# Attention, mixture of experts and feed-forward on one core: three tiles of the last stage taken into the last expert, and the first weight splits in other iterations

## The reference, cut to what matters

```python
# windowed attention, B=4, H=8, S=576, head size 64; window of 64 keys
scores = scale * q @ k.T, masked to 0 <= i - j < 64;  attn = softmax(scores);  x = attn @ v      # x: 2304 x 512
# mixture of experts: 8 experts, 512 -> 1024 -> 512, two per token
noisy = x @ w_gate + log1p(exp(x @ w_noise)) * noise
top2, weights = two largest of noisy, softmax over the two
for e in range(8):
    for k in range(2):
        mask = top2[:, k] == e
        h = maximum(x[mask] @ w1[e], 0)
        out[mask] += weights[mask, k] * (h @ w2[e])
# dense feed-forward, 512 -> 2048 -> 512
h = out @ w_in;  g = h * clip(h + 3, 0, 6) / 6;  result = g @ w_out
```

## Time and profile before

| | us |
|---|---|
| median of 3 runs (1078.79 to 1080.82) | 1079.85 |
| the profiled execution's own time | 1081.28 |
| its span, first to last instruction | 1079.5 |
| PE busy | 1010.3 (94%) |
| DVE, ACT, POOL busy | 418.8, 232.1, 414.5 |

### The profile page before, as it was taken

How to read it: one execution, slowest core, us unless ns; L and a number is a source line. 1 busy time by engine, 2 the same in 40 slices (tenths; PEclk the granted TensorE clock), 3 DMA queues, 4 the chain that set the end, 5 groups by cost and what they waited for, 6 DMA issues and landing times.

```text
span 1079.5 us, 20340 instructions
## 1 busy us (share of the span) xinstructions
PE 1010.3 (94%) x8098; PEld 895.0 (83%) x8099; DVE 418.8 (39%) x885; ACT 232.1 (22%) x537; POOL 414.5 (38%) x277
## 2 busy tenths in 40 slices
PE   6889847999999999999999976999999999999998
PEld 5657727998989999999999966898988988899897
DVE  3477764222213122222222134544545445444333
ACT  4547610111111111111111121111111111211111
POOL 3343469858291928375573817400100101000000
PEclk9989967999999999999999996999999999999999
DMA  8658447936171624435242313310110101100000
GB/s 198 159 140 214 147 161 260 319 123 203 57 224 65 186 100 157 144 106 195 85 159 79 123 63 126 89 30 30 42 48 19 39 29 39 49 1 1 30 1 30
DMA packets 105177, 115.21 MB, mean 107 GB/s; under 512 B 27552, under 2 KB 72608, under 8 KB 105120
## 3 DMA queue, kind: packets, MB, share of 16 engines
q1 hardware_dynamic: 86784, 74.04, 23.5%
q10 hardware_dynamic: 12576, 21.50, 5.7%
q0 software_dynamic: 5760, 18.88, 5.4%
HBM read 76.13 MB, written 38.27 MB: 106 GB/s over the span
## 4 chain that ended last, share of the span: by engine, by line
PE 88%; DVE 6%; issue 2%; SPq 1%; DMA 1%; POOL 1%; ACT 1%; ACTq 0%; DVEq 0%; POOLq 0%
PE PS L1459 21%; PE PS L1443 21%; PE PS L1560 19%; PE PS L1544 19%; PE PS L1328 2%; PE PS L1427 2%; PE PS L1307 1%; PE PS L1291 1%; PE PS L1248 1%; SPq L446 1%; DVE negmax L926 1%; PE PS L1533 1%; DMA k_raw<-in_k_dram 1%; PE PS L1340 1%; PE PS L1269 0%
## 5 line engine op out<-in xcount | busy, mean ns | idle before, releaser
L1459 PE MATMUL PS<-W,hs_room 128*128 128x512 f32 x960 | 246.8, 401 | 4.1 <-DVE hs_room L1071 4.1
L1443 PE MATMUL PS<-xs,W 128*128 128x256 f32 (+1 forms) x1536 | 249.0, 313 | 1.5 <-DVE xs L1065 1.5
L1443 PEld LDWEIGHTS PS<-xs,W 128*128 128x128 f32 x1536 | 239.5, 190 | 12.3 <-issue 2.4
L1560 PE MATMUL PS<-W,gs 128*128 128x512 f32 x864 | 217.4, 396 | 3.6 <-issue 2.5
L1544 PE MATMUL PS<-x2s,W 128*128 128x384 f32 x1152 | 218.9, 339 | 1.5 <-DVE x2s L1168 1.5
L1544 PEld LDWEIGHTS PS<-x2s,W 128*128 128x128 f32 x1152 | 203.4, 190 | 9.0 <-issue 1.9
L610 POOL TENSOR_TENSOR W<-stage,ones_f 128x1024 fp32r<-128x1024 f32 x76 | 144.7, 1903 | 166.9 <-PE PS L1459 156.2
L1459 PEld LDWEIGHTS PS<-W,hs_room 128*128 128x128 f32 x960 | 175.9, 190 | 37.9 <-DVE hs_room L1071 4.5
L1071 DVE SCALAR_TENSOR_TENSOR hs_room<-PS,hs_room 128x256 fp32r<-128x256 f32 (+1 forms) x128 | 62.8, 491 | 333.4 <-ACT hs_room L783 333.2
L1560 PEld LDWEIGHTS PS<-W,gs 128*128 128x128 f32 x864 | 160.9, 188 | 36.0 <-issue 5.8
L612 POOL TENSOR_TENSOR W<-stage,W 128x1024 fp32r<-128x1024 f32 x76 | 181.9, 2393 | 6.0
(11 more groups left out here) (134 smaller groups left out, 580.0 us busy)
## 6 DMA issues: line engine op xcount, KB each, us to landing
stage<-in_moe_w_dram SPq DMA_DIRECT2D x64, 512.0 KB, 4.4
x_in<-x_sorted ACTq DMA_DIRECT2D x40, 256.0 KB, 5.0
x_sorted<-zeros SPq DMA_DIRECT2D x8, 1280.0 KB, 7.5
y_sorted<-y_sb ACTq DMA_DIRECT2D x40, 256.0 KB, 2.1
vD<-in_v_dram SPq DMA_DIRECT2D x72, 64.0 KB
out_dram<-o_sb SPq DMA_DIRECT2D x18, 256.0 KB, 2.2
stage<-in_moe_w_in_dram SPq DMA_DIRECT2D x8, 512.0 KB, 3.9
stage<-in_moe_w_out_dram SPq DMA_DIRECT2D x8, 512.0 KB, 3.6
```

Source lines behind the costliest of these rows:

```text
L1443: last = nc.tensor.matmul(HP_[:, c % 2, 0:n], W[:, par, 0, b, at:at + P], xs[:, a, kd, rows], start=start, stop=(kd == KD - 1 and (a, b) = ...
L1459: last = nc.tensor.matmul(Y[:, first + t, :], hs[:, c % 2, a, t * P:(t + 1) * P], W[:, par, 1, b, c * DM:(c + 1) * DM], start=(c == 0 and ...
L1560: last = nc.tensor.matmul(OP[:, tt, :], gs[:, c % 2, a, tt * P:(tt + 1) * P], W[:, 1, c // FC, b, at:at + DM], start=(c == 0 and (a, b) == ...
```

## The change

Four edits.

- The order in the last expert. Its second part now also prepares tiles 0, 1 and 2 of the last stage: POOL gathers them as soon as blocks 0 to 2 of the last expert and everything older are stored; DVE mixes them after its c = 4, 5, 6; PE turns them after `hidden(5)`, `hidden(6)`, `hidden(7)` (`LAST_AT`); ACT and DVE split them behind that. The gathers of tiles 3, 4, 5 move ahead of POOL's splits of `w_out`. These three tiles always have their rows of the last expert in its blocks 0 to 2.
- The results of part 0, in every expert: DVE copies blocks 0 and 1 before `h_lo(0)` and block 2 behind it; ACT stores 0 and 1 after `h_hi(0)` and 2 after `h_hi(1)`.
- Buffers. `xs` and `x2s` are each two tensors now, laid so that the new ones use rooms that are free in time; `hidden2(0)` has a new wait (`more_moved`), since it writes where the branch of a sixth block would.
- Attention. `FIRST_AT` and `SPLIT_AT`: chunk 3 is loaded after iteration 7 instead of 5 and split in 9 instead of 7; chunk 4 is split in 13 instead of after the loop; later chunks follow.

```diff
+    LAST_AT = (5, 6, 7)
-    FIRST_AT = (2, 3, 4, 5, 7, 9, 11, 13)
-    SPLIT_AT = (4, 5, 6, 7)
+    FIRST_AT = (2, 3, 4, 7, 9, 11, 12, 13)
+    SPLIT_AT = (4, 5, 6, 9, 13)
...
-            split_first(QCH)
+            split_first(QCH + 1)
...
-            for c in range(QCH + 1, SCH):
+            for c in range(QCH + 2, SCH):
...
-            for j in range(BLOCKS):
-                pool.wait_ge(y_stored[j], 16 * (E + 1))
-            pool.wait_ge(more_stored, 16 * (MORE * E + 1))
-
...
+            for j in range(BLOCKS):
+                pool.wait_ge(y_stored[j], 16 * (E + 1) if j < PARTS[1][0] else 16 * E)
+            pool.wait_ge(more_stored, 16 * (MORE * (E - 1) + 1))
             for T in range(GT):
                 gather(T)
 
             expert_done(E - 1)
+            for j in range(PARTS[1][0], BLOCKS):
+                pool.wait_ge(y_stored[j], 16 * (E + 1))
+            pool.wait_ge(more_stored, 16 * (MORE * E + 1))
+            for T in range(GT, 2 * GT):
+                gather(T)
             for c in range(QCH, SCH):
                 pool.wait_ge(stage_full[c % STAGES], 16 * (2 * (E + 1) + 2))
                 split(1, c, (E + 1) * SCH + c - QCH, (E + 1) * SCH + c - QCH + 1)
-            for T in range(GT, TILES):
+            for T in range(2 * GT, TILES):
                 gather(T)
...
-                    if 1 <= c <= PARTS[0][1]:
-                        store_y(e, c - 1, base)
+                    for j in ((0, 1), (2,))[c] if c < 2 else ():
+                        store_y(e, j, base)
...
+                    if c in LAST_AT and last:
+                        x2_hi(LAST_AT.index(c), LAST_AT.index(c), 0)
...
+                move_y(e, 0)
+                move_y(e, 1)
                 for c in range(FC):
                     h_lo(e, 1, c)
-                    if c < PARTS[0][1]:
-                        move_y(e, c)
+                    if c == 0:
+                        move_y(e, 2)
                     if c in TURN_AT[1] and not last:
                         x_lo(e + 1, TURN_AT[1].index(c))
+                    if last:
+                        if c in LAST_AT:
+                            x2_lo(LAST_AT.index(c), LAST_AT.index(c), 0)
+                        if c + 1 in LAST_AT:
+                            mix(LAST_AT.index(c + 1), LAST_AT.index(c + 1))
...
+                        if part == 1 and c in LAST_AT and last:
+                            transpose_x2(LAST_AT.index(c), LAST_AT.index(c))
...
-            for tt in range(GT):
-                transpose_x2(tt, tt, OP[:, tt, :])
             pe.wait_ge(w_ready, SCH * (E + 1))
+            pe.wait_ge(more_moved, MORE * E + 1)
             hidden2(0, 0, 0)
```

More of the change, by code:

```diff
@@ L414, in if_more, with x_place @@
                     eng.sem_inc(signal, each * MORE)
+        def x_place(j, a):
+            part = 0 if j < PARTS[1][0] else 1
+            at = (j - PARTS[part][0]) * P
+            return xs[part][:, a, :, at:at + P]
         def unit(e, part, c):
@@ L1083, in move_y, with mix, x2_lo @@
                 nc.vector.tensor_copy(y_sb[:, j % 3], Y[:, j, :]).then_inc(y_moved, 1)
+            def mix(T, tt):
+                gi = T // GT if isinstance(T, int) else None
+                dve.wait_ge(g_full[tt], 32 * (gi if gi is not None else T[1]) + 32)
+                Tn = T if gi is not None else T[0]
+                nc.vector.tensor_scalar(ya[:, tt, :], ya[:, tt, :], gate[:, 0, bass.ds(Tn, 1)], None, ALU.mult)\
+                    .then_inc(mix_a, 1)
+                dve.wait_ge(mix_a, Tn + 1)
+                nc.vector.scalar_tensor_tensor(yb[:, tt, :], yb[:, tt, :], gate[:, 1, bass.ds(Tn, 1)], ya[:, tt, :],
+                                               ALU.mult, ALU.add).then_inc(x2_ready, 1)
+            def x2_lo(T, tt, par):
+                at = slice(tt * P, (tt + 1) * P)
+                dve.wait_ge(x2hi, T + 1)
+                nc.vector.tensor_tensor(x2s[par][:, 1, :, at], XTP.rearrange("p (k n) -> p k n", k=KD),
+                                        x2s[par][:, 0, :, at].bitcast(F32), ALU.subtract).then_inc(x2_split, 1)
             def more_block(e, t):
@@ L1199, in _ @@
                     .then_inc(out_ready, 1)
[L1200 to L1203, removed]
-            x2_lo(GT - 1, GT - 1, 0, OP[:, GT - 1, :])
             with dve.Fori(0, GPAIRS - 1) as gp:
@@ L1432, in hidden @@
                 first, blocks = PARTS[part]
-                rows, n = slice(first * P, (first + blocks) * P), blocks * P
+                n = blocks * P
                 if c == 0:
@@ L1442, in hidden @@
                     for a, b in PASSES:
-                        last = nc.tensor.matmul(HP_[:, c % 2, 0:n], W[:, par, 0, b, at:at + P], xs[:, a, kd, rows],
+                        last = nc.tensor.matmul(HP_[:, c % 2, 0:n], W[:, par, 0, b, at:at + P], xs[part][:, a, kd, :],
                                                 start=start, stop=(kd == KD - 1 and (a, b) == PASSES[-1]))
@@ L1498, in more_block, with transpose_x2 @@
                 last.then_inc(more_y, 1)
+            def transpose_x2(T, tt):
+                pe.wait_ge(x2_ready, T + 1)
+                pe.wait_ge(x2_split, T + 1)
+                for kd in range(KD):
+                    last = nc.tensor.transpose(XTP[:, kd * P:(kd + 1) * P], yb[:, tt, kd * P:(kd + 1) * P], ident[:])
+                last.then_inc(t2_full, 1)
             def expert(e, par, last=False):
@@ L1508, in expert @@
                         hidden(e, par, part, c)
-                        if c in TURN_AT[part]:
-                            j = TURN_AT[part].index(c)
-                            if part == 0:
-                                turn_x(e, PARTS[1][0] + j)
-                            elif not last:
-                                turn_x(e + 1, j)
+                        if part == 0 and c in TURN_AT[0]:
+                            turn_x(e, PARTS[1][0] + TURN_AT[0].index(c))
+                        if part == 1 and c in TURN_AT[1] and not last:
+                            turn_x(e + 1, TURN_AT[1].index(c))
+                        if part == 1 and c in LAST_AT and last:
+                            transpose_x2(LAST_AT.index(c), LAST_AT.index(c))
                         project(e, par, part, c - 1)
@@ L1526, in _ @@
             expert(E - 1, 1, last=True)
-            def transpose_x2(T, tt, bank=XTP):
-                pe.wait_ge(x2_ready, T + 1)
-                if bank is XTP:
-                    pe.wait_ge(x2_split, T + 1)
-                for kd in range(KD):
-                    last = nc.tensor.transpose(bank[:, kd * P:(kd + 1) * P], yb[:, tt, kd * P:(kd + 1) * P], ident[:])
-                last.then_inc(t2_full, 1)
             def hidden2(gi, c, par):
```

46 lines of the change are left out of this document (16 added, 30 removed).

## The result

The changed kernel takes 1068.68 us (median of 4 runs, 1066.27 to 1070.30) where the kernel before takes 1079.62 (now 4 runs, 1078.79 to 1080.82): a ratio of 0.9896, 95% interval 0.9873 to 0.9919. Faster by 10.9 us, 1.0%; forecast were 16.1. Its profiled execution took 1067.66 for a span of 1065.9.

A forecast was written before the change was run, and what follows sets the result against it. It took PE to bound the kernel, with time to gain only in PE's gaps. Transition 11.7 (14.5 - 0.4 - 2.4) plus attention 4.4 made 16.1, so 1079.85 - 16.1 = 1063.8 us; own range 1061 to 1066, whole range 1060 to 1069.

The forecast's parts named there:

- Three turns, 1.08, and a stall of 0.4: Last expert: three turns inside it end it 1.08 us later; PE's waiting for mixes and splits adds 0.4 (bounds 0 and 1.5).
- The third rival: Last expert stalls: late gathers or a longer mix chain hold `h_lo(5)` to `h_lo(7)` and `project`; 1068 to 1070; chance 0.13.
- Gathers in time: Last expert: gathers start near 624.1; tile 0's second lands at 629.1, 0.8 us before its first mix.
- First `project2` behind the splits: Transition: `g_chain(0)` waits for splits of `w_out`, so `project2` starts at 651.45, gaining 14.5 less 0.4; PE ready 4.4 earlier.
- The clock falls again, 2.4: Before the first `project2`: the 4.4 us wait drops PE's clock for 4.8 us of work, losing 2.4 (bounds 0 and 3.0).
- The first rival: Before the first `project2`: the clock stays up through the 4.4 us wait; 2.4 us less, 1061.4; chance 0.16.
- New order of results, 0: All eight experts: copying and storing the results in the new order costs 0, covered by PE's work.
- Attention, 4.4: Attention: 3.7 gained in iteration 7 plus 1.0 from a wait of PE, less 0.3 for moved splits.
- the moved splits: Attention, iterations 9 and 13: splits placed there cost 0.3 us for both (bounds 0 and 4.8).
- the wait without a releaser: Attention, 54.59 to 56.70: PE's 2.11 us loss while chunk 3 loads; moving the load gains 1.0 (bounds 0 and 2.1 and the clock's share).
- The second rival: Attention: splits only move their damage; `nsp` held in 9 and 13, 2 x 2.4 eat 3.7 + 1.0; 1068.2; chance 0.16.
- One sign of being wrong: Attention: the prediction would be wrong if iterations 9, 10, 13 or 14 grow beyond 6.6 us.

The follow-up runs named there:

- last_only: The changed kernel with the old tables FIRST_AT and SPLIT_AT: 1072.75 us, ratio 0.9929 to the kernel before.
- room64: The changed kernel with the experts' region's base rounded to 64 bytes, so xs and x2s begin at multiples of 64: 1062.44 us, ratio 0.9830 to the kernel before.
- before_store_order: The kernel before with only the new order of `move_y` and `store_y` in every expert: 1092.93 us against 1093.92, ratio 0.9997.
- attn_only: The kernel before with only the new tables FIRST_AT and SPLIT_AT: 1075.64 us against 1080.66, ratio 0.9955.
- fill: The changed kernel with 20 unread matmuls between the first two `hidden2` groups: 1068.07 us, ratio 0.9884 to the kernel before.
- g_first: The changed kernel with the first `g_chain` behind one split of `w_out` instead of four: 1061.96 us, ratio 0.9826 to the kernel before.
- g_first_room64: The changed kernel with both edits, of g_first and of room64: 1055.72 us, ratio 0.9770 to the kernel before.
- x2s_off32: The kernel before with all tensors of its last stage 32 bytes further on: 1085.82 us against 1080.66, ratio 1.0044.
- before_room64: The kernel before with the region's base rounded to 64, which there moves only the experts' tiles: 1077.15 us against 1080.27, ratio 0.9966.

## Why the prediction was right, and where it was too large

- **Three turns, 1.08, and a stall of 0.4.** The expert ended at 635.36, which is 641.61 in before's times (its second part starts 6.25 earlier); forecast 641.42 without the stall. No stall: its lower bound, 0, holds. The third rival falls.
- **Gathers in time.** Forecast start 624.1, measured 618.48 + 6.25 = 624.7. From the last store's issue to the gather it took 3.7 us, not 2.8. The first mix didn't wait, but of the margin of 0.8 little was left: the second gather of the tile was issued at 619.80, which with the 3.7 of the earlier trace rows is 623.5, and the mix began at 623.56.
- **First `project2` behind the splits.** Forecast 651.45 in before's times, measured 651.57; gain to there 14.1 forecast, 14.39 measured. PE ready 4.4 us early: it was 4.92, as `hidden2` started 0.6 sooner than the branch was costed.
- **The clock falls again, 2.4.** It fell, 3.7 us after PE went idle, and stood at 0.50 for 5.6 us of `project2` and `hidden2`. It cost 2.5 in after, 2.3 in last_only and 1.3 in room64: mechanism and size are right. What the sum lacks is the wait behind it for DVE operations that POOL's splits hold: 0.6 in after (0.38 of it idle), 1.4 in room64. Clock and waits together, 3.15 and 2.75, are 0.75 and 0.35 above the 2.4. The first rival (the clock stays up) falls.
- **New order of results, 0.** before_store_order: no difference that it can tell.
- **Attention, 4.4.** Measured 5.0 by attn_only and 4.56 between the copies of 7 and 15. Its parts came out otherwise: iteration 7 gave 3.73 (3.7 forecast), the moved splits cost 0.2 (0.3), and the wait without a releaser didn't go (1.0 forecast, 0 found): the load of chunk 3 wasn't its cause, and what is, stays open. The 1.0 was made good by another thing, iteration 8, which gave 1.06, as the low clock behind the long wait of 7 was gone with it. That the sum of 4.4 fits is luck by this much. The second rival falls: `nsp` at 79.86 came ahead of the low split that would have held it. The Trainium skill's rule, "SBUF — State Buffer", section "Who interferes with whom", did show elsewhere: the trace agrees at 654.08 (a DVE operation with two SBUF inputs, 2.69 us and not 0.56, issued 0.11 after POOL's split) and in fill (2.61 and not 0.75). One sign of being wrong that the prediction names did come, 9 and 13 at 7.3, beyond 6.6. The sign was badly chosen: it goes by POOL's copy, which now stands behind the split, and each next iteration gave the time back.
- **The step that failed** is one that the prediction doesn't have: that the last stage runs at its old pace behind the first `project2`. The buffers moved `x2s` to another region, and its place cost 3.89 us. The forecast of 1063.8 with this and the 0.75 of clock and waits is 1068.4; measured 1068.68, nearer than the interval of 2.5 us to a side can tell. The sum's own range, 1061 to 1066, missed. That the result lies in the whole range, 1060 to 1069, is luck: its upper end came from two rivals, splits that only move their damage (1068.2) and stalls in the last expert (1068 to 1070), and neither happened.

## What to carry to other kernels

When a change moves an operand to other memory, compare its start address before and after, also where nothing about the work differs: 3.9 us in one stage and 3.4 in another, 0.7% together, lay in 32 bytes. When a large wait is taken away, list what PE reaches next and whether its maker lies beside another engine's long SBUF work; in fill, g_first, g_first_room64 and room64 PE came to the fourth tile's turn earlier and found a wait of 1.0 to 2.0 us there, until POOL's splits were put behind the mix. And weigh a wait by whether the clock falls in it: the waits of 1.5 us cost themselves, those of 4.9 us cost themselves and 1.3 to 2.5 more.

## What the runs showed of the hardware that I had not expected

- **A matmul's moving operand that starts 32 bytes off a multiple of 64 is slower.** 12 matmuls of 384 fp32 columns take 2.12 us instead of 2.09 (340 and 337 ns each), a group of 24 in the experts 4.40 instead of 4.33. Shown in both directions in `x2s` (x2s_off32, room64) and by moving `xs` (before_room64). Only offsets of 0 and 32 were tried. In these runs other tensors moved with them, but the hidden products' other operand, `W`, stayed. `project2`, whose moving operand is `W`, changed by 0.01 in 2.10; whether that comes from its other operand, `gs`, which moved too, isn't shown.
- **PE's clock.** The same wait of 4.9 to 5.0 us ahead of `project2` had different costs. In after the clock fell 3.7 us after PE's last matmul and came back 5.6 us after work began again; in room64 it was 4.6 and 3.0, in before, with the longer idle stretch, 3.3 and 4.8. It stayed at 1.00 through waits of 1.40, 1.52 and 1.59. In fill it fell 2.6 us after PE stopped for a wait of 2.03, when PE was at work again; before that wait PE had worked for 19 us. And of the wait of 2.1 in attention, the clock fell behind it in before (56.8) and stayed up in after. What tells these cases apart the runs don't show.
- **POOL's splits hold DVE's operations whose inputs all lie in SBUF until a split ends**: the two of the mix take 2.12 and 2.61 us and not 0.48 and 0.75 (the first has one tensor and one number per row as inputs, the second two tensors), the last of `g_chain` 2.69 and not 0.56. Operations that read PSUM aren't held: in after, the `hc` at 652.35 takes 0.56 beside the split that POOL began at 652.00.
